# Prologue order, GpSimd's share of the chunk products, and the TensorE order of a fused attention and MLP kernel

## The reference

```python
def _attn_ref(r, k, v, w, u):            # B, H, S, D = 2, 8, 768, 48
    state = np.zeros((B, H, D, D))
    for t in range(S):
        kt, vt, rt, wt = (k[:, :, t], v[:, :, t], r[:, :, t], w[:, :, t])
        cur = np.einsum('bhd,bhe->bhde', u[None] * kt, vt)
        y[:, :, t] = np.einsum('bhd,bhde->bhe', rt, state + cur)
        state = wt[:, :, :, None] * state + np.einsum('bhd,bhe->bhde', kt, vt)

def _moe_ref(x, mu_k, mu_r, w_k, w_v, w_r):      # x: (2, 768, 384), d_ff 1024
    x_prev = x shifted by one step
    xk = mu_k * x + (1.0 - mu_k) * x_prev
    xr = mu_r * x + (1.0 - mu_r) * x_prev
    k = np.maximum(xk @ w_k, 0.0)
    return sigmoid(xr @ w_r) * (k * k @ w_v)

def _moe2_ref(x, w_in, g_ln, w_sg, b_sg, w_out):
    h = gelu(x @ w_in);  u, v = halves of h
    v_n = layer_norm(v) * g_ln
    v_s = np.einsum('ts,bsd->btd', w_sg, v_n) + b_sg[None, :, None]
    return x + (u * v_s) @ w_out
```

## Time and profile before

| | |
|---|---|
| median of 3 runs | 343.54 us |
| profiled execution | 342.36 us |
| its span | 340.6 us |
| mean granted TensorE clock | 0.98 of full speed |
| TensorE matmul busy | 314.1 us, 2658 instructions |
| VectorE busy | 205.6 us |
| ScalarE busy | 148.5 us |
| GpSimd busy | 136.0 us |

### The profile page before, as it was taken

The page is one execution under the profiler, slowest core; times in us unless marked ns, Lnnn a source line. Parts: engine busy times, 40 slices in busy tenths (PEclk is TensorE's granted clock), DMA queues, the critical chain, the costliest instruction groups (busy, mean ns, idle before and its releaser), DMA issues.

```text
span 340.6 us, 6668 instructions
## 1 busy us (share of the span) xinstructions
PE 314.1 (92%) x2658; PEld 298.0 (87%) x2658; DVE 205.6 (60%) x295; ACT 148.5 (44%) x280; POOL 136.0 (40%) x111
## 2 busy tenths in 40 slices
PE   0850999999999999999999999999999999999996
PEld 0740988989998999999999999899999988999996
DVE  4989858798299559937922536694543637214431
ACT  4243573644545284346445495574211315411100
POOL 7478587136434333522323033276133107512320
PEclk9995799999999999999999999999999999999999
DMA  7939104404402240400004107200000120000012
GB/s 248 409 118 392 77 2 163 160 2 162 162 3 76 89 159 3 163 7 2 2 8 167 72 0 279 92 3 0 0 2 0 69 71 1 0 2 0 2 46 92
DMA packets 11281, 28.14 MB, mean 83 GB/s; under 512 B 1264, under 2 KB 6000, under 8 KB 9968
## 3 DMA queue, kind: packets, MB, share of 16 engines
q1 hardware_dynamic: 10272, 25.40, 21.2%
q10 hardware_dynamic: 976, 2.30, 1.8%
HBM read 24.74 MB, written 2.36 MB: 80 GB/s over the span
## 4 chain that ended last, share of the span: by engine, by line
PE 85%; DVE 7%; issue 3%; ACT 2%; DMA 1%; POOL 0%; ACTq 0%; DVEq 0%
PE pm L282 16%; PE pm L283 15%; PE pm L284 15%; PE py L679 3%; PE ps L603 3%; PE ps L284 3%; PE ps L283 3%; PE ps L282 3%; PE pkt L628 3%; PE py L666 3%; DVE suffix L1086 2%; DVE xf L1144 2%; PE pkt L284 2%; PE pkt L283 2%; PE pu L284 2%
## 5 line engine op out<-in xcount | busy, mean ns | idle before, releaser
L526 POOL TENSOR_TENSOR k_l<-sq,k_h 128x512 fp32r<-128x512 f32 x24 | 32.7, 1361 | 58.7 <-ACT sq L907 58.7
L282 PE MATMUL pm<-xkr_h,wk_h 128*128 128x256 f32 x144 | 41.8, 291 | 0.0
L282 PE MATMUL pm<-k_h,wv_h 128*128 128x256 f32 x144 | 40.8, 284 | 0.4 <-POOL k_l L526 0.4
L283 PE MATMUL pm<-k_l,wv_h 128*128 128x256 f32 x144 | 40.7, 283 | 0.0
L284 PE MATMUL pm<-k_h,wv_l 128*128 128x256 f32 x144 | 40.7, 283 | 0.0
L283 PE MATMUL pm<-xkr_l,wk_h 128*128 128x256 f32 x144 | 40.7, 283 | 0.0
L284 PE MATMUL pm<-xkr_h,wk_l 128*128 128x256 f32 x144 | 40.7, 282 | 0.0
L514 POOL TENSOR_TENSOR r_in<-inw,prod 128x512 f32<-128x512 f32 x12 | 15.4, 1285 | 49.4 <-issue 29.7
L585 POOL TENSOR_TENSOR gated_l<-gf,gated_h 128x384 fp32r<-128x384 f32 x16 | 16.4, 1024 | 46.5 <-ACT gated_h L1018 36.2
L1144 DVE SCALAR_TENSOR_TENSOR xf<-X,omu,xf 128x256 f32<-128x256 f32 x36 | 22.3, 672 | 14.1 <-ACT xf L867 14.1
L899 ACT ACTIVATE relu<-pm 128x512 f32<-128x512 f32 x24 | 14.3, 595 | 37.5 <-PE pm L284 37.5
(11 more groups left out here) (232 smaller groups left out, 885.5 us busy)
## 6 DMA issues: line engine op xcount, KB each, us to landing
inw<-in_units SPq DMA_DIRECT2D x10, 1026.5 KB, 5.0
vb<-in_vT SPq DMA_DIRECT2D x12, 256.0 KB, 5.1
wsg_raw<-in_wsgT SPq DMA_DIRECT2D x1, 2304.0 KB, 8.3
out_y<-y_out SPq DMA_DIRECT2D x12, 192.0 KB, 1.9
wk_raw<-in_moe_w_k ACTq DMA_DIRECT2D x3, 512.0 KB, 12.1
wv_raw<-in_moe_w_v SPq DMA_DIRECT2D x4, 384.0 KB, 6.9
win_raw<-in_moe_w_in SPq DMA_DIRECT2D x3, 512.0 KB, 4.9
inw<-in_units SPq DMA_DIRECT2D x2, 512.0 KB, 5.3
```

The source lines that it names most:

```text
L282: pe.matmul(o, a_h, b_h, start=first and n == 0, stop=False, skip_group_check=True)
L283: pe.matmul(o, a_h, b_l, start=False, stop=False, skip_group_check=True)
L526: pool.tensor_tensor(k2_l[:, 2 * n:2 * n + 2], sq[:, j % 2].rearrange("p (g t) -> p g t", g=2), k2_h[:, 2 * n:2 * n + 2], ALU.subtract).th ...
```

## The change

In words, by engine:
- VectorE: `scan` now also makes r_in, behind k_in. In the prologue omu comes before mask(0), carry_on(0) before mask(1), both bonuses behind mask(1), with output(0) between them; then the low part of the second w_k piece, choose(0) and mix(0), and only then carry_on(1), scan(2) and scan(3). In a stage the mask of unit b comes before scan(a+2), and the mask of unit a+2 before the next choice.
- GpSimd: `scaled` becomes `products`, only rkp, behind a wait for r_in. It begins when both first r_in are done; the low part of w_k[2] waits for the end of mix(0).
- TensorE: in a unit from_state comes before add_state (`outputs`); the scores of the next unit stand right behind the outputs of one (in stages 1 to 4), the transposes a tile later; the scores and transposes of the next stage's first unit stand before and between its value tiles.
- ScalarE no longer issues weights; keys(0) stands behind the cast of w_r, and the keys of a stage's first unit behind the mixing of the stage before.
- SP issues w_r and the first w_k piece after v(0), the other two after vf(1), before unit 2.
- `part_split` counts the pieces that GpSimd and VectorE split apart.

```diff
--- before.py
+++ after.py
@@ -288,22 +288,23 @@
...
         WSPLIT += [("wv", wv_raw, wv_h, wv_l, 2 * n, 2 * n + 2) for n in range(4)]
-        POOLED = len(WSPLIT)
         WSPLIT += [("win", win_raw, win_h, win_l, kt, kt + 1) for kt in range(KT)]
...
+        POOLED = [j for j, x in enumerate(WSPLIT) if x[0] in ("wr", "wv") or (x[0] == "wk" and x[4] != 1)]
         def parts_of(name):
...
             eng.wait_ge(wh_done, j + 1)
-            if j < POOLED:
-                eng.wait_ge(wl_done, j + 1)
-            else:
-                eng.wait_ge(wl2_done, j + 1 - POOLED)
+            pooled = sum(x <= j for x in POOLED)
+            eng.wait_ge(wl_done, pooled)
+            if j + 1 > pooled:
+                eng.wait_ge(wl2_done, j + 1 - pooled)
...
@@ -444,9 +445,14 @@
...
             load_v(0)
+            wk = parts_of("wk")
+            load_part(sp, 0)
+            load_part(sp, wk[0])
             load_vf(0)
...
             load_vf(1)
+            load_part(sp, wk[1])
+            load_part(sp, wk[2])
             load_unit(2)
...
@@ -500,22 +506,13 @@
...
-            def scaled(un):
-                wu = inw[:, un % 3]
-                ru, ku = wu[:, W1:W1 + WIDE], wu[:, W1 + WIDE:W1 + 2 * WIDE]
-                if un < 2:
-                    pool.wait_ge(s_rk[un], 16)
-                else:
-                    pool.wait_ge(s_in[un % 3], 16 * (un // 3 + 1))
-                pool.wait_ge(prod_done, un + 1)
-                if un >= 2:
-                    pool.wait_ge(y_mm, un - 1)
-                pool.tensor_tensor(blocks(r_in[:, un % 2]), blocks(ru), prod[:, un % 2, :, 0:C],
-                                   ALU.mult).then_inc(rin_done, 1)
+            def products(un):
+                pool.wait_ge(rin_done, un + 1)
                 if un >= 2:
                     pool.wait_ge(c_mm, un - 1)
-                pool.tensor_tensor(rkp[:, un % 2], ru, ku, ALU.mult).then_inc(rkp_done, 1)
+                pool.tensor_tensor(rkp[:, un % 2], inw[:, un % 3, W1:W1 + WIDE],
+                                   inw[:, un % 3, W1 + WIDE:W1 + 2 * WIDE], ALU.mult).then_inc(rkp_done, 1)
...
@@ -527,31 +524,33 @@
...
             wk, wv = parts_of("wk"), parts_of("wv")
-            scaled(0)
-            scaled(1)
+            pool.wait_ge(rin_done, 2)
+            products(0)
+            products(1)
             low_part(pool, 0, wl_done)
             low_part(pool, wk[0], wl_done)
-            scaled(2)
-            low_part(pool, wk[1], wl_done)
+            pool.wait_ge(xl_done, KT)
             low_part(pool, wk[2], wl_done)
-            scaled(3)
+            products(2)
+            products(3)
             low_part(pool, wv[0], wl_done)
...
             low_part(pool, wv[3], wl_done)
-            scaled(4)
             key_low(0, 2)
+            products(4)
             key_low(0, 3)
-            scaled(5)
+            products(5)
             for s in range(1, STAGES):
+                key_low(s, 0)
                 if 2 * s + 4 < NU:
-                    scaled(2 * s + 4)
-                for n in range(KG):
+                    products(2 * s + 4)
+                for n in range(1, KG):
                     key_low(s, n)
                 if 2 * s + 5 < NU:
-                    scaled(2 * s + 5)
+                    products(2 * s + 5)
...
@@ -714,17 +713,23 @@
...
+            def outputs(un):
+                bonus(un)
+                from_state(un)
+                add_state(un)
+                from_chunk(un)
             scores(0)
             keys_by_step(0)
+            add_state(0)
+            scores(1)
             bonus(0)
-            add_state(0)
+            from_chunk(0)
+            from_state(1)
+            from_chunk(1)
             bonus(1)
-            scores(1)
-            from_chunk(0)
             keys_by_step(1)
             flag_of(0)
-            from_state(1)
-            from_chunk(1)
             add_state(1)
...
@@ -734,40 +739,34 @@
...
                     first_mlp(s, *KS[1])
-                    bonus(a)
-                    add_state(a)
-                    from_state(a)
-                    from_chunk(a)
+                    outputs(a)
                     scores(b)
...
                     first_mlp(s, *KS[2])
-                    bonus(b)
-                    add_state(b)
-                    from_state(b)
-                    from_chunk(b)
-                    for tile in KS[3:] + VS:
-                        first_mlp(s, *tile)
+                    outputs(b)
+                    first_mlp(s, *KS[3])
+                    scores(b + 1)
+                    first_mlp(s, *VS[0])
+                    keys_by_step(b + 1)
+                    first_mlp(s, *VS[1])
                 elif s < STAGES - 1:
-                    scores(a)
-                    keys_by_step(a)
                     first_mlp(s, *RS[0])
-                    bonus(a)
-                    add_state(a)
-                    from_state(a)
-                    from_chunk(a)
+                    outputs(a)
+                    scores(b)
                     first_mlp(s, *RS[1])
+                    keys_by_step(b)
                     first_mlp(s, *KS[0])
-                    scores(b)
-                    keys_by_step(b)
                     flag_of(s + 1)
                     first_mlp(s, *KS[1])
-                    bonus(b)
-                    add_state(b)
-                    from_state(b)
-                    from_chunk(b)
-                    for tile in KS[2:] + VS:
+                    outputs(b)
+                    if b + 1 < NU:
+                        scores(b + 1)
+                    for tile in KS[2:] + VS[:1]:
                         first_mlp(s, *tile)
+                    if b + 1 < NU:
+                        keys_by_step(b + 1)
+                    first_mlp(s, *VS[1])
                 else:
...
@@ -918,16 +917,13 @@
...
             check(0)
-            for j in [0] + wk:
-                load_part(act, j)
             check(1)
+            high_weight(0)
             keys(0)
-            high_weight(0)
-            high_weight(wk[0])
+            for j in wk:
+                high_weight(j)
             keys(1)
             flag_out(0)
-            high_weight(wk[1])
-            high_weight(wk[2])
             act.wait_ge(s_par, 16)
...
@@ -949,18 +945,20 @@
...
                     mix(s + 1)
+                    keys(b + 1)
                 elif s < STAGES - 1:
-                    keys(a)
+                    gate(s, *RS[0])
                     check(a)
-                    gate(s, *RS[0])
                     check(b)
                     gate(s, *RS[1])
+                    keys(b)
                     key_high(s, 0)
-                    keys(b)
                     flag_out(s + 1)
...
                     mix(s + 1)
+                    if b + 1 < NU:
+                        keys(b + 1)
                 else:
...
@@ -1072,7 +1070,6 @@
...
                 if un >= 2:
-                    dve.wait_ge(rin_done, un - 1)
                     dve.wait_ge(state_done, states(un - 1))
...
@@ -1094,6 +1091,10 @@
...
                                   ALU.mult).then_inc(kin_done, 1)
+                if un >= 2:
+                    dve.wait_ge(y_mm, un - 1)
+                dve.tensor_tensor(blocks(r_in[:, p]), blocks(inw[:, un % 3, W1:W1 + WIDE]), prod[:, p, :, 0:C],
+                                  ALU.mult).then_inc(rin_done, 1)
...
@@ -1184,35 +1185,39 @@
...
             scan(1)
+            dve.wait_ge(s_par, 16)
+            dve.tensor_scalar(omu[:], mu, -1.0, 1.0, ALU.mult, ALU.add).then_inc(omu_done, 1)
             dve.wait_ge(s_att, 1)
             mask(0)
-            bonus(0)
             carry_on(0)
             mask(1)
+            bonus(0)
+            output(0)
             bonus(1)
-            output(0)
             output(1)
-            carry_on(1)
-            dve.wait_ge(s_par, 16)
-            dve.tensor_scalar(omu[:], mu, -1.0, 1.0, ALU.mult, ALU.add).then_inc(omu_done, 1)
-            scan(2)
+            low_part(dve, parts_of("wk")[1], wl2_done)
             choose(0)
...
             mix(0)
+            carry_on(1)
+            scan(2)
             scan(3)
...
                 if s < STAGES - 1:
-                    mask(a)
+                    if s == 0:
+                        mask(a)
                     bonus(a)
...
                     output(a)
+                    mask(b)
                     if a + 2 < NU:
                         scan(a + 2)
-                    mask(b)
                     bonus(b)
...
                     output(b)
+                    if a + 2 < NU:
+                        mask(a + 2)
                     choose(s + 1)
...
```

## The result

The changed kernel takes 337.23 us, median of 4 runs (336.88 to 337.48), against 343.49 for the kernel before in the same comparison (342.80 to 343.79): ratio 0.982, 95% interval 0.9803 to 0.9837. A second comparison gave 337.00 against 343.49, ratio 0.9825 (0.9803 to 0.9847). The forecast was 339.2 with a range of 334.8 to 342.8. The profiled execution took 336.88, its span is 335.2 where that of before was 340.6. So it is faster by 1.8%, as forecast and clear of the noise, and by 2 us more than forecast.

The account below looks back on a forecast made before the run. The end was taken as the first MLP matmul's start plus later stalls plus the work behind. Terms -7.0 + 1.7 - 0.6 + 2.2 + 0.2 and -0.9 + 0.1 gave -4.3 us: 339.2, range 334.8 to 342.8.

Parts of the forecast that it names:

- The start: Prologue: undisturbed scans bring mask(0) to 12.3 and scores(1) to 13.8; y of unit 1 done at 21.5 against 21.90.
- rival D: Prologue: w_r lands after 11.3 and delays all that follows; slower, 344.9 us if it lands at 17; chance 0.08.
- their 7.03: Start of stage 0: the clock falls again, so r and the first k tile keep their slow 7.03 us.
- Choice and mixing first: Before stage 0: mixing ahead of scan(2) starts the first MLP matmul at 27.4 against 34.41, 7.0 us earlier.
- The stall before scores(2): Stage 0: state product waits for GpSimd's w_k[2], then scan(2) takes 4.0; TensorE stalls 1.7 us, 5.3 of 7.0 left.
- The stall before scores(4): Stage 0: scan(4), stretched by GpSimd's queue, ends at 55.8; TensorE, there at 53.6, stalls 2.2 us.
- Steady stages: After stage 0: unit order saves 0.18 per unit, 0.9 us for five units; excursions to small matmuls cost 0.1.
- The sum: Whole kernel: -3.5 and -0.8 make -4.3 us, 338.1 from the profiled execution; 339.2 against the median.
- four signs of being wrong: w_r landing after 11.3, y later than 22, no scan(4) operation stretched, or TensorE waiting in a steady stage.
- B: Stage 0: VectorE gets in between GpSimd's operations, so both stalls are absent; 335.3 us; chance 0.2 with its halves.
- C: Stage 0: the clock falls in a stall (+1.6) or the choice reaches ScalarE late; 340.3 to 342.5 us; chance 0.18.
- E: Stage 0: late w_v and key lows slip over 4 us behind scan(4); within 0.2% of 343.5; chance 0.09.

Follow-up runs that it names:

- e1: The changed kernel, but GpSimd splits the low part of w_k[2] right behind w_k[0], without waiting for the first mixing; 335.24 us.
- e5: The changed kernel with carry_on(1) and scan(2) again ahead of the low part of w_k[1], the choice and mixing of stage 0; 338.19 us.
- e6: The changed kernel with the 62 filler matmuls of e4 and the early low part of w_k[2] of e1; 334.97 us.
- e7: e1 with scores(4) and keys(4) behind the first value tile, mask(4) behind stage 1's mixing, the last key low ahead of products(4); 335.31 us.
- e9: e7 with bonus(3), carry_on(3) and output(3) in front of scan(4) on VectorE in stage 0; 334.42 us, repeated at 334.21.
- e2: The changed kernel with the old TensorE order inside a unit: bonus, add_state, from_state, from_chunk; 337.99 us.
- e3: The changed kernel with scores, transposes, masks and keys of stages 1 to 4 back at their old places, new unit order kept; 338.03 us.
- e4: The changed kernel with 62 unread identity matmuls on TensorE: 20 before scores(0), 8 before add_state(0), 34 behind add_state(1); 338.13 us.
- e10: e9 with 13, 5 and 20 filler matmuls on TensorE; 335.84 us.

## Why the prediction was right, and where it was off

**What bounds it.** Right: the end is the first MLP matmul, plus stalls, plus the work behind. The three columns of the table are this sum.

**The start (forecast 27.4, measured 28.93).** scan(0) and scan(1) fell to their undisturbed lengths, mask(0) at 12.20 against 12.3, w_r was there at 11.28 against 11.0 (rival D's point was 11.3, so it was near), scores(1) at 14.02 against 13.8 (mask(0) was done at 13.54; add_state(0), at half pace, ended at 14.02). Then a step failed: "Behind scores(1) (1.1) come ... about 1.03 each". scores(1) took 2.01 and bonus(0) 1.34, and y was done at 23.13 instead of 21.5. I had taken the length from the trace of before, where scores(1) run at 16.16 and the engine was at its full clock (its first record starts at 13.72); in the new order they come 2.1 us earlier, in time that is still at 1.2 GHz in this trace (first record at 16.73). e1 shows the step as I meant it: scores(1) 1.09, y done at 21.51, first MLP matmul 27.30. Missed in the same way was that the gate tiles and the first k tile would keep their 7.03: without the stall they took 7.82, for the clock rose 4.9 us after the first MLP matmul and not 3.2. The granted clock of the changed kernel:

```profile
26.50:27.00 0.50, 0.00 (x0) 0.00 (x0) 0.50 (x2) 0.50 (x2) 0.00 (x0) 0.97 0.86 345
27.00:33.00 6.00, 4.07 (x18) 4.06 (x19) 5.88 (x10) 2.99 (x7) 1.97 (x1) 0.50 1.02 385
33.00:34.00 1.00, 1.00 (x8) 1.00 (x7) 1.00 (x2) 0.74 (x2) 0.40 (x1) 0.60 1.17 437
```

**Choice and mixing first.** From the end of y to the copy or clearing of X 2.77 (forecast 2.7) and from there to the end of the first low part 2.88 (forecast 3.05). The mechanism and its size held. e5 shows what the prediction only implied: of the 3.4 us that it brings, 1.2 remain.

**The stall before scores(2).** The mechanism held, and so did its size: the state was done 2.74 us after the end of the mixing (30.95 to 33.69; forecast 29.3 to 32.1) and scores(2) started 4.05 behind it (forecast 4.0). The state product's own length was 2.37 where the prediction's signs say "some 1.7". The stall was smaller, 0.99 against 1.7, because TensorE lost the 0.8 of the clock as well and reached scores(2) at 36.75. Of the 5.3 that were to be left there, 3.70 were.

**The stall before scores(4).** All four operations of scan(4) are stretched; it ended at 56.31 against 55.8. TensorE was there at 54.91 and not at 53.6, so the stall was 1.50 against 2.2. Stage 1 started 3.14 earlier; forecast 3.5. The large miss at the start had mostly been cancelled: 1.5 of a late first MLP matmul and 0.8 of the clock, less 0.7 and 0.7 of stall that this lateness hid, and less some 0.5 that is left over and lies in and around units 2 and 3, beyond the 0.4 forecast there. That stage 1 came within 0.4 of its forecast is therefore in part luck. e6 shows the reverse, an early TensorE that had to wait again (1.51 before scores(4)). e7 and e9 show what the stall was worth: nothing by itself, because the mixing was next (e7 against e1); 2.3 us of "between" for e9 against the changed kernel once output(3) and w_k[2] were moved too.

**Steady stages (forecast 0.8, measured 2.3).** The term mis-sized most. I counted two pairs of equal shape at 0.09 each, 0.18 per unit. It was 0.30 per unit (e2), since all four operations got shorter: bonus by 0.10, add_state by 0.09, from_state by 0.05, from_chunk by 0.04. And I had costed the new places of scores and transposes at +0.1, by counting excursions from the MLP matmuls. Together they brought 0.85 (e3); that scores directly behind from_chunk save more than a transpose between MLP matmuls costs is my reading, not a run of its own. The Trainium skill, "TensorEngine Tiling (Array Packing)", Key Properties, says that a change of tiling mode drains TensorE. The trace agrees as far as it goes: a group is shorter beside a group of its own shape (bonus 0.92 against 1.02, add_state 0.52 against 0.61). That draining is the reason no run here shows. The prediction used the rule to count three more excursions against the change, and by e3 the new places gained all the same. TensorE waited in no steady stage more than before: 0.38 in stage 5 in both traces.

**The sum.** By spans 5.4 us were gained, 4.3 forecast: 0.4 less until stage 1, 1.5 more behind it. The other 0.9 of the miss in the median lies in the base. The profiled execution of before was among its short ones (342.36 where the median was 343.54) and I carried that 1.2 over; the changed kernel's profiled execution lies 0.35 below its median. So a near hit in the time hides two large misses of opposite sign, 1.5 at the start and 1.5 in the steady stages.

**The signs.** Of the four signs of being wrong one came true: y was to be written by 22 and was at 23.13. It did tell of a real miss, the clock in the first matmuls. The other three did not: w_r landed by 11.28, scan(4) was stretched, and TensorE waits in no steady stage that it did not wait in before.

**The rivals.** B (the stalls are absent): no, but both were smaller. C: no in this kernel (the granted clock stays at 1.00 behind both stalls), yes in e4. E: no, GpSimd's key lows were done at 60.1, ahead of TensorE's use. D: no, but w_r came only just in time, 11.28 where the point was 11.3.

## What to carry to other kernels

When two vector engines share operands in SBUF, put the second one's work beside the first one's PSUM operations, and look for the one operation that gates a consumer: one GpSimd operation in the wrong place made a VectorE operation of 0.42 us last 2.37 (e1). When something large is moved forward, follow each engine until it next waits: of 3.4 us gained at the start of the first MLP, 2.2 were given back at two later waits (e5), and removing a wait pays only if the next dependency has been moved as well (e7 against e9). On TensorE, group small matmuls by tile shape and put them next to each other; together with the new places of the transposes this gave 2.3 us in stages 1 to 4.

Before a length is carried over from a trace, ask at which clock it was taken and whether the clock will be the same at the new place; and where a view reads full clock, check against the length of a known instruction.

## What the runs showed of the hardware that I had not expected

- A wait of TensorE inside a busy stretch can cost more than its length: after 1.90 us of idle (e4) and 1.85 (e10) the granted clock went to 0.50 for some 3 us, 1.1 and 1.8 us after TensorE had begun again (3.50 us for a k tile instead of 2.32, e4); after 0.99, 1.50 (after) and 1.60 (e1) it did not.
- TensorE's first matmuls run at the lower clock level, which the view of the granted clock does not show because the trace has no record there; the change to full clock came between 11.7 and 19.7 us in the eleven traces without fillers and at 6.6 to 8.1 in the three with them. It moves the first MLP matmul by 1.6 us between kernels with the same beginning (27.30 in e1, 28.93 after).
- Two chains of operations that read SBUF twice double each other: 4.0 us of scan(4) became 8.8, and GpSimd's 768-column low parts went from 1.9 to 2.3 to 2.75.
